# One low part and one piece moved in VectorE's order, one load moved in SyncE's queue

## The reference, cut to what matters

```python
# attention: 4 batches x 8 heads, 576 positions, head dim 64, mask by blocks of 64
scores = scale * np.matmul(q, k.transpose(0, 1, 3, 2))
scores = np.where(block_i >= block_j, scores, -1e9)
attn = softmax(scores)                 # row maximum, exp, divide by sum + 1e-9
x = attn @ v                           # -> [2304, 512] tokens by model width
# gated layer, width 1536
gate = 1.0 / (1.0 + np.exp(-(x @ w_gate)))
x = gate * (x @ w_val) @ w_out         # [2304, 512]
# four experts, width 1024, mixed by normalised domain_probs
p = domain_probs / (domain_probs.sum(-1, keepdims=True) + 1e-09)
for e in range(4):
    out += p[:, e:e+1] * (np.maximum(x @ w1[e], 0.0) @ w2[e])
```

## Time and profile before

| what | value |
|---|---|
| median of 3 runs | 1462.43 us (1461.35 to 1463.72) |
| profiled execution | 1460.69 us, of which the span 1458.9 us |
| TensorE, matmuls busy | 1412.2 us (97% of the span) |
| VectorE busy | 899.9 us (62%) |
| ScalarE busy | 727.1 us (50%) |
| GpSimd busy | 432.2 us (30%) |
| granted TensorE clock | 0.995 of full speed over the span |

### The profile page before, as it was taken

How to read it: one execution, slowest core, us unless ns; L and a number is a source line. 1 busy time by engine, 2 the same in 40 slices (tenths; PEclk the granted TensorE clock), 3 DMA queues, 4 the chain that set the end, 5 groups by cost and what they waited for, 6 DMA issues and landing times.

```text
span 1458.9 us, 22264 instructions
## 1 busy us (share of the span) xinstructions
PE 1412.2 (97%) x7816; PEld 1285.4 (88%) x7816; DVE 899.9 (62%) x1551; ACT 727.1 (50%) x1472; POOL 432.2 (30%) x675
## 2 busy tenths in 40 slices
PE   5998998999999999999999999999999999999999
PEld 4877777899998989899999989899899999899897
DVE  4887889677545546376774636364757646364453
ACT  4777888656444324254663535253546436243341
POOL 3555667544201212021541112021234312022100
PEclk8999999999999999999999999999999999999999
DMA  7787887122214122132232222131232312131302
GB/s 167 187 205 179 212 217 183 50 81 77 83 32 143 58 73 73 44 97 77 73 89 86 87 73 73 44 102 44 73 97 63 101 58 73 44 102 44 101 8 80
DMA packets 201198, 136.76 MB, mean 94 GB/s; under 512 B 66144, under 2 KB 170624, under 8 KB 201088
## 3 DMA queue, kind: packets, MB, share of 16 engines
q1 hardware_dynamic: 199504, 134.42, 33.2%
q10 hardware_dynamic: 1520, 0.89, 0.3%
q0 software_dynamic: 64, 0.04, 0.0%
HBM read 97.55 MB, written 9.44 MB: 73 GB/s over the span
## 4 chain that ended last, share of the span: by engine, by line
PE 84%; DVE 8%; SPq 3%; DMA 2%; issue 1%; ACT 1%; POOL 1%; DVEq 0%; ACTq 0%; POOLq 0%
PE pb L929 26%; PE pb L931 25%; PE pb L930 25%; DVE ptl L335 2%; PE pt L400 2%; SPq L146 2%; DVE nmax L313 2%; PE ov L425 1%; PE st L388 1%; PE st L436 1%; SPq L138 1%; PE st L389 1%; DVE x1p L348 1%; DMA craw<-in_moe_w_dram 1%; DVE qtl L341 1%
## 5 line engine op out<-in xcount | busy, mean ns | idle before, releaser
L929 PE MATMUL pb<-xch,ul 128*128 128x384 f32 x1176 | 398.7, 339 | 5.2 <-DVE cb L863 3.7
L931 PE MATMUL pb<-xch,uh 128*128 128x384 f32 x1176 | 393.6, 335 | 0.0
L930 PE MATMUL pb<-xcl,uh 128*128 128x384 f32 x1176 | 393.3, 334 | 0.0
L720 POOL TENSOR_TENSOR us<-ura 128x256 f32<-128x256 f32 x84 | 62.3, 742 | 850.7 <-DVE ul L664 832.6
L929 PEld LDWEIGHTS pb<-xch,ul 128*128 128x128 f32 x1176 | 220.7, 188 | 23.1 <-issue 16.1
L931 PE MATMUL pb<-ch,rh 128*128 128x512 f32 x576 | 224.6, 390 | 0.0
L930 PE MATMUL pb<-cl,rh 128*128 128x512 f32 x576 | 224.5, 390 | 0.0
L929 PE MATMUL pb<-ch,rl 128*128 128x512 f32 x576 | 224.1, 389 | 0.0
L930 PEld LDWEIGHTS pb<-xcl,uh 128*128 128x128 f32 x1176 | 220.9, 188 | 0.4
L931 PEld LDWEIGHTS pb<-xch,uh 128*128 128x128 f32 x1176 | 220.7, 188 | 0.0
L832 DVE TENSOR_TENSOR cl<-craw,ch 128x512 fp32r<-128x512 f32 x132 | 91.5, 707 | 113.8 <-ACT ch L767 113.6
(11 more groups left out here) (104 smaller groups left out, 2553.6 us busy)
## 6 DMA issues: line engine op xcount, KB each, us to landing
ura<-in_moe_w_dram SPq DMA_DIRECT2D x96, 256.0 KB, 3.1
craw<-in_moe_w_dram SPq DMA_DIRECT2D x96, 256.0 KB, 2.8
ura<-in_moe_w_gate_dram SPq DMA_DIRECT2D x36, 256.0 KB, 3.3
ura<-in_moe_w_val_dram SPq DMA_DIRECT2D x36, 256.0 KB, 3.3
craw<-in_moe_w_out_dram SPq DMA_DIRECT2D x36, 256.0 KB, 3.2
qhl<-qth SPq DMA_DIRECT2D x32, 144.0 KB, 3.2
qhl<-qtl SPq DMA_DIRECT2D x32, 144.0 KB, 3.1
qlh<-qtl SPq DMA_DIRECT2D x32, 144.0 KB, 3.1
```

The costliest lines, as they stand in the source:

```text
L720: nc.gpsimd.tensor_tensor(us[:, 0, :], a21, a22, ALU.add).then_inc(us_ok, 1)
L929: nc.tensor.matmul(acc, lhs[1], rhs[0], start=start, stop=False, skip_group_check=True)
L930: nc.tensor.matmul(acc, lhs[0], rhs[1], start=False, stop=False, skip_group_check=True)
L931: return nc.tensor.matmul(acc, lhs[0], rhs[0], start=False, stop=stop, skip_group_check=True)
```

## The change

Three moves of existing work; no instruction is added or taken away.

1. `dve_unit`: where the predecessor is a val unit, lo_4 of unit n+1 is issued behind C12 of unit n and no longer between gated_21 and hidden_lo. In all other units its place is the same.
2. SyncE: `load_xb` is issued in turn 14 of a pass, behind that turn's `load_unit`, and no longer in turn 13, ahead of the first two pieces of w2.
3. At the end of the gated units VectorE takes the low part of the second w_out piece behind C22 of unit 11 and no longer ahead of it.

```diff
@@ dve_unit
             if before and kind(n - 1) == "up":
                 r21(n - 1)
-            if more:
-                lo_4(dve, n + 1)
             if before and kind(n - 1) == "val":
                 hidden_lo(n - 1)
+            elif more:
+                lo_4(dve, n + 1)
             c11(n)
             c12(n)
+            if before and kind(n - 1) == "val" and more:
+                lo_4(dve, n + 1)
             if before and kind(n - 1) == "up":
                 r_rest(n - 1)
@@ SyncE
-                    if j == 2 * GUNITS + 1 and s + 1 < SUPERS:
+                    if j == 2 * GUNITS + 2 and s + 1 < SUPERS:
                         sp.wait_ge(x_lo, XSPLITS * (2 * s + 1))
                         load_xb(sp, s + 1)
@@ VectorE
                 for j in range(0 if s else 2, 2 * GUNITS):
                     dve_unit(n0 + j)
-                    if j >= 2 * GUNITS - 2:
-                        lo_piece(c0 + j - 2 * GUNITS + 2)
+                    if j == 2 * GUNITS - 2:
+                        lo_piece(c0)
                 c22(n0 + 2 * GUNITS - 1)
+                lo_piece(c0 + 1)
                 gated_rest(n0 + 2 * GUNITS - 1)
```

## The result

The changed kernel takes 1470.28 us (median of 8 runs, 1468.40 to 1473.75), the kernel before 1461.31 us (8 runs, 1458.12 to 1463.72): ratio 1.0068, 95% interval 1.0058 to 1.0079, so 0.6 to 0.8% slower. 1463.2 was forecast, with a range up to 1466.2; the time lies outside it. The profiled execution has a span of 1469.7 us, against 1458.9.

What follows compares the result with a forecast made beforehand. TensorE, busy 97% of the span, was taken as the bound. Parts 1, 2 and 3 gave +2.3 - 1.5 + 0 = +0.8 us on the 1462.43 us median: 1463.2 us, range 1460.2 to 1466.2 us.

Steps and rivals of the forecast that it cites:

- What bounds the kernel: TensorE, busy 97% of the span; in gate units its product 4 already waits for VectorE's C22, 0.20 us over the pitch.
- Part 1 on VectorE: lo_4 ahead of C22 in gate units: 0.34 us price less 0.19 us, 0.15 us per unit, 15 times, +2.3 us.
- relief of 0.19: In gate units hidden_lo takes 1.89 us instead of 2.08, as GpSimd's third sum ends about 0.19 us earlier.
- exclusive lock: VectorE and GpSimd share a port pair; whoever comes second is blocked entirely, making hidden_lo's gain 0.20 us.
- Part 2: Tokens' load behind w2's first pieces: removes the 1.51 us stall at product 4, first pass only; -1.5 us, bounds -1.5 to +1.5.
- Part 3: At the projection, C22 of unit 11 ahead of the second piece's low part: zero, bounds -0.2 to +0.3 us.
- what else waits for lo_4: SyncE's load of unit n+3, issued at about 698.3 instead of 694.11, complete at about 701.8: cost nothing.
- The margin: Some 0.2 us between the end of GpSimd's four sums, about 704.8, and VectorE's gated_rest at 704.89 + 0.15.
- Rival B: Late load of unit n+3 makes gated_rest wait for GpSimd, delaying product 7: 12 x 0.6 us, 1470.4 us; chance 0.08.
- point of decision: gated_rest must wait if the load of unit n+3 lands more than 3.7 us after its first issue, 0.2 us extra latency.

Runs made afterwards that it cites:

- e5: Changed kernel with three buffers for raw block 4 and lo_4 of a gate unit's successor moved behind C22 of unit n: 1455.56 us, ratio 0.9967.
- e6: As e5, with the low parts of each projection's first two pieces also behind C22: 1449.60 us, ratio 0.9930.
- e3: Kernel before, with SyncE waiting in gate units for C12 of unit n before issuing the load of unit n+3: 1467.17 us, ratio 1.0043.
- e8: Kernel before with 128 empty instructions on TensorE at its start: 1458.80 us, ratio 0.9997.
- e10: Kernel before with 64 extra small matmuls on TensorE at its start: 1462.65 us, ratio 1.0019.
- e1: Kernel before with only lo_4 moved behind C12 in gate units; token load and piece order as before: 1472.77 us, ratio 1.0084.
- e7: Changed kernel with 128 empty instructions on TensorE at its start: 1469.54 us, ratio 1.0064.
- e9: Changed kernel with 64 extra small matmuls on TensorE at its start: 1474.80 us, ratio 1.0095.
- e11: Changed kernel with lo_4 of a gate unit's successor moved behind C22 and the load still tied to it: 1475.79 us, ratio 1.0106.
- e4: Changed kernel with three buffers for raw block 4 and three transfers per load, which no longer waits for lo_4 of unit n+1: 1460.12 us, ratio 1.0000.

## Why the prediction was wrong, point by point

- *What bounds the kernel*: right. TensorE stood still for C22 in gate units, and in e5 and e6 what came earlier there came off the time.
- *Part 1 on VectorE*: right, also in size. lo_4 takes 0.42 us at its new place, the second sum 0.74 instead of 0.93, hidden_lo 1.90 instead of 2.08, and product 4 is 0.16 us later against a forecast of 0.15. e5 confirms the relief of 0.19 from the other side. On the exclusive lock that the prediction cites, the trace agrees that the later one waits, but not to the recorded end: hidden_lo is 0.32 us longer where 0.47 us of the third sum's record were left, and 0.14 us longer (1.90) where 0.28 us were left. The rows decide: the wait is shorter than that rule makes it.
- *Part 2*: the mechanism is right, and the 1.5 us came in the executions compared. But the stall that was to go is no fixed one. Among the other kernels with the tokens' load at its old place, TensorE idles there for 1.7 us in e3, 1.2 in e8 and 0.35 in e10, not at all in e1, and e10 has 1.36 us at the same place of the second pass (840.6), where the forecast saw no gain.
- *Part 3*: no effect of its own was looked for; with part 2 it gained 2.2 us, against 1.5 forecast, and the interval (0.9 to 3.8 us) holds both.
- **The step that failed** is the one on what else waits for lo_4: "Two transfers are issued some 0.5 us apart and land in 3.0 to 3.4 us: complete at about 701.8. ... The margin is some 0.2 us: cost nothing". The issue did move by the 4.2 us, and eight of 12 loads did land within 3.4 us and cost nothing. Two terms were mis-sized. The landing: one row from a quiet stretch stood for all 12 loads, and one load in three had its second transfer land at 4.8 to 5.0 us, 1.5 us later, with an instruction fetch in it; the profile had shown the fetches only as a queue with 0.3% of the time. The margin: of rows 11, 3.0 us is the first transfer and 3.4 the second, counted from its own issue 0.4 us later, so the load is complete at 698.3 + 0.4 + 3.4 = 702.1 and not 701.8, and the first sum begins 0.2 us behind the landing. By the prediction's own rows the fourth sum then ends some 0.2 us behind gated_rest's start, and so it does; that is harmless. The margin that counted was the 0.5 to 0.7 us by which the fourth sum starts ahead of gated_rest, and the late landing is more than that.
- In the trace before none of this was to be seen on these 12 loads: no fetch stands in their first 4 us, and all land within 3.6 us. They also had room: the load issued at 694.11 was complete at 697.9, and its first sum waited for lo_s until 700.48. Over the whole trace the same line shows how long a landing can be:

```profile
DMA to landing us min/median/max: 2.4/3.2/6.3
```

- *Rival B* named the late load and 1470.4 us. Its total is right by chance: I priced 12 collisions at 0.6 us, by way of gated_rest and product 7. There were 4, at 2.4 us each, by way of ScalarE. Its point of decision, 3.7 us from the first issue, was wrong too: eight loads complete at 3.6 to 3.9 us cost nothing, the four at 5.2 to 5.4 us cost all. In these each engine pushed the other once more (1.86, 1.23 and 1.05 us in the rows above), line 644 needs all four sums, and s1b is queued behind it. A wait moved onto an engine's queue costs all that stands behind it there. B had a chance of 0.08; a margin thinner than the scatter of what it rests on should have had it near even.

## What to carry to other kernels

Moving an instruction moves what its semaphore lets go: here the operation cost 0.16 us in each gate unit, some 2 us in sum, and the buffer that it freed later cost some 10 us. Before a load's issue is moved later, count the landing of its last transfer from the first issue, compare the margin left with the longest landing of that line in the whole trace and not with the median of one stretch, and count the instruction fetches among the traffic: a fetch that misses a load before the move can fall into it after. Where two engines hold each other up, ask which comes first: the fourth sum ahead of gated_rest cost nothing, behind it more than a microsecond. If the release is the trouble, a third buffer for only the piece that is released late (here 1 KB a partition) was enough, and the reordering could then be pushed further.

## What the runs showed of the hardware

- One 16 KB fetch of TensorE's instructions (63 in a run) that begins 2.1 to 3.1 us after the first issue of a load of two times 256 KB puts the second landing from about 3.3 to between 4.4 and 5.2 us (20 loads of this kind in six runs: after, e1, e3, e7, e9, e11). Three that began 0.8 to 1.2 us after it (e11) went with 3.9 to 4.5 us. That the load's last share waits on one DMA engine while the others are done is in the rows above; that it is the engine that did the fetch is my reading, for the trace doesn't name the engine.
- Behind one of the four stalls of the changed kernel, TensorE went on at half speed for some 3 us: ten starts in a row 0.32 us apart. The granted clock in 4 us behind the stall at 347.75, and behind that at 711.39 (PEclk is the column before the last but one; 0.57 and 1.00 of 2.4 GHz, so mostly the lower level of 1.2 GHz in the first):

```profile
348.50:352.50 4.00, 4.00 (x16) 4.00 (x15) 2.42 (x3) 2.49 (x3) 3.68 (x4) 0.57 0.00 0
711.00:715.00 4.00, 3.60 (x20) 3.46 (x21) 2.45 (x3) 3.31 (x6) 2.53 (x4) 1.00 0.00 0
```

Both stalls are alike (2.38 and 2.18 us idle). It cost 1.6 us once; e1, e3, e7, e9 and e11 show it after one or two of their stalls too, the kernel before and e4 nowhere. In the layers' part of all profiled executions it stands behind 9 of the 17 stalls of 2.18 to 3.47 us and behind none of the 17 of 1.06 to 1.75 us. Why one stall brings it and the next doesn't stays open.
- Why e1_part1 loses more than the changed kernel and its 1.5 us (12.3 against 10.5 us) stays within the two intervals and was not followed up; its six times lie in two groups, 1470.0 to 1470.3 and 1475.3 to 1476.6 us.
